# First stretch and routing of a fused attention, expert layer and MLP rebuilt together

## What is computed

```python
# attention, B=2, H=8, S=768, D=64: window |i-j| < 16 and, beside it, 24 block summaries
k_sum = k.reshape(B, H, nb, 32, D).max(axis=3)
v_sum = v.reshape(B, H, nb, 32, D).mean(axis=3)
scores_l = where(|i-j| < 16, q @ k.T / 8, -1e9)
scores_s = q @ k_sum.T / 8 + log(32)
a = softmax(concat(scores_l, scores_s)) ; attn = a @ concat(v, v_sum)
# expert layer on N=1536 rows x of 512: E=8 experts, F=1024, top-1
logits = x/|x| @ (emb/|emb|).T / tau
idx = argmax(logits) ; gate = softmax(logits)[idx]
out[idx == e] = gate * (relu(x @ w1[e]) @ w2[e])
# second layer
h = relu(x @ w_in)            # 512 -> 2048
result = (h * h) @ w_out      # 2048 -> 512
```

## Time and profile before

| | us |
|---|---|
| median of 3 runs | 585.4 (583.68 to 589.5) |
| the profiled execution | 588.62, its span 586.9 |
| PE busy | 539.4 (92% of the span) |
| DVE busy | 282.1 (48%) |
| ACT busy | 231.7 (39%) |
| POOL busy | 113.0 (19%) |
| mean granted clock of TensorE | 0.956 |

### The profile page before, as it was taken

One profiled execution on the slowest core, in us unless ns is written; L12 is line 12 of the kernel. 1 busy time (PEld: TensorE's weight loads), 2 busy tenths in 40 slices (PEclk: granted clock), 3 DMA queues, 4 the chain that ended last, 5 costly groups with the idle time before them and its releaser, 6 DMA issues.

```text
span 586.9 us, 11035 instructions
## 1 busy us (share of the span) xinstructions
PE 539.4 (92%) x4482; PEld 486.2 (83%) x4482; DVE 282.1 (48%) x437; ACT 231.7 (39%) x405; POOL 113.0 (19%) x134
## 2 busy tenths in 40 slices
PE   7498779499999896899999999999999999999997
PEld 6377667498989795889988989989989999998995
DVE  4667757556788494745747223232223223223321
ACT  4568656165564343443654222222122222212221
POOL 8282110111107789520100000000000000000000
PEclk9689988579999998999999999999999999999999
DMA  5877860893729694857721002002002002000000
GB/s 181 200 203 180 194 173 30 267 348 120 251 75 323 227 333 158 282 178 254 250 92 54 1 1 73 0 1 71 0 0 71 0 0 71 0 0 37 1 1 36
DMA packets 62655, 69.50 MB, mean 118 GB/s; under 512 B 22512, under 2 KB 47088, under 8 KB 62232
## 3 DMA queue, kind: packets, MB, share of 16 engines
q1 hardware_dynamic: 59160, 57.36, 31.6%
q0 software_dynamic: 3456, 11.60, 5.6%
HBM read 58.88 MB, written 10.06 MB: 117 GB/s over the span
## 4 chain that ended last, share of the span: by engine, by line
PE 68%; DVE 9%; DMA 9%; POOL 8%; issue 4%; SPq 1%; ACT 1%; POOLq 0%; DVEq 0%
PE psum L881 20%; PE psum L882 20%; PE psum L883 20%; POOL win_lo L522 3%; DMA v_blk<-in_v 2%; POOL win_hi L520 2%; DMA k_raw<-in_k 2%; DMA x_rows_sb<-x_rows,idx_g 1%; DMA win_raw<-in_moe_w_in 1%; DMA x_rows_sb<-x_rows,gather_tab 1%; DVE neg_max L1308 1%; PE psum L708 1%; PE psum L666 1%; DVE wb_lo L1561 1%; PE psum L726 1%
## 5 line engine op out<-in xcount | busy, mean ns | idle before, releaser
L883 PE MATMUL psum<-x_hi,win_lo 128*128 128x256 f32 x384 | 108.7, 283 | 0.0
L882 PE MATMUL psum<-x_lo,win_hi 128*128 128x256 f32 x384 | 108.7, 283 | 0.0
L881 PE MATMUL psum<-x_hi,win_hi 128*128 128x256 f32 x384 | 108.5, 282 | 0.0
L1652 DVE TENSOR_TENSOR h_sq<-h_relu 128x512 f32<-128x512 f32 x48 | 33.2, 691 | 126.6 <-ACT h_relu L1248 126.6
L881 PE MATMUL psum<-wb_hi,h_hi 128*128 128x512 f32 x208 | 83.2, 400 | 0.0
L883 PE MATMUL psum<-wb_hi,h_lo 128*128 128x512 f32 x208 | 81.8, 393 | 0.0
L882 PE MATMUL psum<-wb_lo,h_hi 128*128 128x512 f32 x208 | 81.7, 393 | 0.0
L1248 ACT ACTIVATE h_relu<-psum 128x512 f32<-128x512 f32 x48 | 28.7, 597 | 127.4 <-PE psum L883 127.4
L881 PEld LDWEIGHTS psum<-x_hi,win_hi 128*128 128x128 f32 x384 | 73.6, 192 | 1.4
L882 PEld LDWEIGHTS psum<-x_lo,win_hi 128*128 128x128 f32 x384 | 73.6, 192 | 1.4
L883 PEld LDWEIGHTS psum<-x_hi,win_lo 128*128 128x128 f32 x384 | 73.6, 192 | 0.0
(11 more groups left out here) (199 smaller groups left out, 926.0 us busy)
## 6 DMA issues: line engine op xcount, KB each, us to landing
w_raw<-in_moe_w SPq DMA_DIRECT2D x56, 512.0 KB, 6.1
win_raw<-in_moe_w_in POOLq DMA_DIRECT2D x8, 512.0 KB, 5.2
w_raw<-in_moe_w_out SPq DMA_DIRECT2D x8, 512.0 KB, 5.1
k_raw<-in_k SPq DMA_DIRECT2D x8, 384.0 KB, 3.6
q_raw<-in_q SPq DMA_DIRECT2D x8, 384.0 KB, 5.5
v_blk<-in_v SPq DMA_DIRECT2D x3, 1024.0 KB, 8.0
v_win<-in_v SPq DMA_DIRECT2D x16, 192.0 KB, 3.9
x_rows<-x_all SPq DMA_DIRECT2D x8, 384.0 KB, 4.7
```

The source lines that it names most:

```text
L881: pe.matmul(o, l_hi, r_hi, start=start, stop=False)
L882: pe.matmul(o, l_hi, r_lo, start=False, stop=False)
L883: return pe.matmul(o, l_lo, r_hi, start=False, stop=stop)
L1652: dve.tensor_tensor(h_sq[c % 2][:, :], h_relu[c % 2][:, :], h_relu[c % 2][:, :], ALU.mult)\
```

## The change

1. **Start.** SP loads the embeddings first, and both `load_near` of slots 0 and 1 ahead of the wait for the means; `load_qk(2)` goes behind the means. DVE clears slots 0 and 1 (POOL keeps 2 and 3). Chunk 0 of v is summed by halving, one half of the chunk on DVE and the other on POOL. POOL makes the mask from one band that it copies. The three `fill` of pair 0 go to three PSUM banks, and their filler matmuls (`keep_warm`, 24 in all) are gone. The embeddings are normalised and turned ahead of the first scores.
2. **Pair steps.** `turn_tile` is gone. In the step of pair n, PE turns all six tiles of pair n-1 (`turn_pair`, into the two banks of the turned exponentials), ACT and DVE move a half each, and the second `turn_probs` waits for both. From the step of pair 1 on, DVE regroups k one step earlier. The squares leave the attention.
3. **Routing.** Logits of batch 0 stand between pairs 4 and 5, the comparison in pair 5, the counting in pairs 5 and 6, the placing in pair 6, the list in pair 7. In pairs 6 and 7 ACT moves both halves of the turned exponentials. The norms leave the choice: the largest logit of a row doesn't depend on the row's norm, so `margin` keeps the differences and is scaled in expert block 2. Batch 1 is weighed in the up part of block 0, counted in its down part and placed in the up part of block 1. The 16 filler matmuls ahead of the first `turn_rows` are gone.
4. **w_in.** POOL splits pieces 0, 1, 6 and 7, ACT and DVE split 2 and 3 at the end of block 2, and 4 and 5 at the end of block 3. Gathers 3 and 4 and scatters 1 and 2 no longer stand behind splits on POOL; gather 5, the first of the loop, stands behind the loads and splits of 6 and 7.

The core of the diff (buffers moved in SBUF, renamed semaphores and the removed helpers are left out):

```diff
--- before.py
+++ after.py
+            sp.dma_start(emb_sb[:, :], emb).then_inc(emb_loaded, 16)
             load_qk(0)
             sp.dma_start(v_blk[:, 0, :], v_blocks[:, 0, :]).then_inc(vb_loaded[0], 16)
-            sp.dma_start(emb_sb[:, :], emb).then_inc(emb_loaded, 16)
-            sp.dma_start(tau_sb[:, 0:1], tau.broadcast_to([P, 1])).then_inc(emb_loaded, 16)
-            load_qk(1)
+            sp.dma_start(tau_sb[:, 0:1], tau.broadcast_to([P, 1])).then_inc(tau_loaded, 16)
             sp.wait_ge(zeros_made, 1)
             load_near(0, 0, free=True)
-            load_qk(2)
+            load_qk(1)
+            sp.wait_ge(zeros_made, 2)
+            load_near(0, 1, free=True)
             sp.wait_ge(mean_made, 1)
             sp.dma_start(mean_dram[0:P, :], v_mean[:, 0, :]).then_inc(means_stored[0], 16)
             sp.dma_start(v_blk[:, 1, :], v_blocks[:, 1, :]).then_inc(vb_loaded[1], 16)
             sp.wait_ge(means_stored[0], 16)
             load_means(0, 0)
             load_means(0, 1)
-            load_near(0, 1, free=True)
+            load_qk(2)
             sp.dma_start(v_blk[:, 2, :], v_blocks[:, 2, :]).then_inc(vb_loaded[2], 16)
             load_qk(3)
-            sp.wait_ge(zeros_made, 2)
+            sp.wait_ge(late_zeros_made, 1)
...
+            pool.wait_ge(vb_loaded[0], 16)
+            pool.wait_ge(consts_made, 1)
+            at = BLOCK * D // 2
+            width = at // 2
+            while width >= D:
+                last = pool.tensor_tensor(v_blk[:, 0, at:at + width], v_blk[:, 0, at:at + width],
+                                          v_blk[:, 0, at + width:at + 2 * width], ALU.add)
+                if width > D:
+                    after(last)
+                width //= 2
+            last.then_inc(half_summed, 1)
...
             scatter(0, scatter_tab0)
+            pool.wait_ge(logits_summed, 2)
+            load_win(0)
+            load_win(1)
+            split_win(0, 1)
+            split_win(1, 2)
             pool.wait_ge(x_stored[1], 16 * PAIRS // B)
             pool.wait_ge(routed, 2)
             nblk, final = block_count(pool)
-            load_win(0, 0)
-            load_win(1, 1)
             gather(3, gather_tab)
-            split_win(0)
-            split_win(1)
+            pool.wait_ge(squares_done, NT)
+            load_win(2)
+            load_win(3)
             scatter(1, scatter_tab0)
-            split_win(2)
             gather(4, gather_tab)
-            split_win(3)
-            split_win(4)
+            load_win(4)
+            load_win(5)
             scatter(2, scatter_tab0)
-            split_win(5)
-            split_win(6)
-            split_win(7)
+            load_win(6)
+            load_win(7)
+            split_win(6, 3)
+            split_win(7, 4)
...
+            def turn_pair(pair, bank=4):
+                for half in range(2):
+                    for t in range(GT):
+                        mm = pe.transpose(psum[:, bank + half, t * P:(t + 1) * P], x_all[:, pair, GT * half + t, :],
+                                          ident[:, :])
+                    mm.then_inc(xt_turned, 1)
+            def wait_turned(pairs):
+                pe.wait_ge(xt_moved[0], pairs)
+                pe.wait_ge(xt_moved[1], pairs)
...
+                if pair > 0:
+                    turn_pair(pair - 1)
                 if fills:
                     fill(it + 1, par, 1)
-                if ahead:
-                    scores(*nxt, 1)
+                if pair > 0:
+                    wait_turned(pair)
+                turn_probs(it, par, 1)
+                scores(*nxt, 1)
                 if fills:
                     fill(it + 1, par, 2)
                 values(it, par, 1)
...
-                fill(0, 0, f, first=True)
-                keep_warm(ps_warm, 5)
+                fill(0, 0, f, first=True, bank=(7, 4, 5)[f])
+            pe.wait_ge(emb_normed, 1)
...
+            pair_step(2, 0, True)
+            logits(4)
+            scores(3, 0, 0)
+            pe.wait_ge(logits_moved, 1)
+            turn_probs(2, 1, 0)
+            fill(3, 1, 0)
+            values(2, 1, 0)
+            turn_logits(0, 5)
+            fill(3, 1, 1)
+            pe.wait_ge(logits_read, 1)
+            turn_probs(2, 1, 1)
+            scores(3, 0, 1)
+            fill(3, 1, 2)
+            values(2, 1, 1)
             pe.wait_ge(consts_made, 2)
-            totals(0, 7)
-            values(it, 0, 1)
-            turn_probs(it, 1, 0)
+            totals(0, 5, at=GT * P)
+            turn_pair(4)
+            scores(3, 1, 0)
+            wait_turned(5)
+            pe.wait_ge(totals_moved, 1)
+            turn_probs(3, 0, 0)
             pe.wait_ge(before_made, 1)
+            pe.wait_ge(qk_moved_act, 2 * PAIRS)
             ranks(0, 7)
-            values(it, 1, 0)
-            turn_probs(it, 1, 1)
+            values(3, 0, 0)
...
+            def weigh_second(c):
                 if c == 0:
...
+                    turn_pair(PAIRS - 1, bank=6)
+                elif c == 1:
+                    wait_turned(PAIRS)
+                    logits(6)
+                elif c == 2:
+                    turn_logits(1, 7)
+            def count_second(t, f):
+                if (t, f) == (0, 0):
+                    totals(1, 0)
+                elif (t, f) == (0, 3):
+                    ranks(1, 1)
...
+            def place_second(c):
+                if c == 2:
                     pe.wait_ge(y_moved_dve, 1)
-                    ranks(1, 5)
-            def place_second(t, f):
+                    slots(1, 5)
...
-            keep_warm(psum[:, 3, :], 16)
             turn_rows(0, bank=0)
...
+                if squared is not None:
+                    for t in range(squared, squared + TILES):
+                        squares(t)
+                if win is not None:
+                    win_hi_part(win)
+                    win_hi_part(win + 1)
...
                 scale_out(it, par, 0)
+                if pair > 0:
+                    move_pair(pair - 1)
                 if fills:
                     move_kq(it + 1, par)
                 move_prob(it, par, 1)
                 if fills:
                     key_max(it + 1, par)
-                if ahead:
-                    row_max(*nxt, 1)
-                if tile is not None:
-                    move_tile(tile + 1)
+                if 0 < pair < PAIRS - 3:
+                    regroup_k(*((it + 1, 1) if par == 0 else (it + 2, 0)))
+                row_max(*nxt, 1)
...
+            def move_pair(pair, bank=4):
+                dve.wait_ge(xt_turned, 2 * pair + 2)
+                dve.tensor_copy(x_t1[:, pair % KC, GT * P:2 * GT * P], psum[:, bank + 1, 0:GT * P])\
+                   .then_inc(xt_moved[1], 1)
...
+            def sum_blocks():
+                dve.wait_ge(vb_loaded[0], 16)
+                width = BLOCK * D // 4
+                while width >= D:
+                    link(dve.tensor_tensor(v_blk[:, 0, 0:width], v_blk[:, 0, 0:width], v_blk[:, 0, width:2 * width],
+                                           ALU.add))
+                    width //= 2
+                dve.wait_ge(half_summed, 1)
+                at = BLOCK * D // 2
+                dve.tensor_tensor(v_mean[:, 0, :], v_blk[:, 0, 0:D], v_blk[:, 0, at:at + D], ALU.add)\
+                   .then_inc(mean_made, 1)
...
             regroup_k(0, 0, first=True)
-            move_kq(0, 0, first=True)
+            embeddings()
+            move_kq(0, 0, first=True, bank=4)
             dve.wait_ge(key_zeros_made, 1)
             key_max(0, 0)
+            dve.wait_ge(emb_zeros_made, 1)
+            dve.wait_ge(emb_turned, 1)
+            dve.tensor_copy(emb_t[:, :, 0:E], ps_emb.rearrange("p (c e) -> p c e", e=E)).then_inc(emb_moved, 1)
+            row_max(0, 0, 0)
+            sum_blocks()
+            row_max(0, 0, 1)
             regroup_k(0, 1, first=True)
-            row_max(0, 0, 0)
-            row_max(0, 0, 1)
-            block_means(0)
...
+            choose(0, 5)
+            move_kq(3, 1)
+            move_prob(2, 1, 1)
+            key_max(3, 1)
+            row_max(3, 0, 1)
+            scale_out(2, 1, 1)
+            move_pair(4)
+            move_totals(0, 5, at=GT * P)
+            row_max(3, 1, 0)
             lay_blocks(0, 7)
+            scale_out(3, 0, 0)
             place(0, 7)
+            row_max(3, 1, 1)
             make_hots(0)
-            scale_out(last, 1, 0)
+            scale_out(3, 0, 1)
             list_tokens(0, 7)
-            move_prob(last, 1, 1)
-            scale_out(last, 1, 1)
+            scale_out(3, 1, 0)
...
+            expert(1, behind=place_second)
+            expert(2, behind=lambda c: scale_margins() if c == 0 else None, win=2)
+            expert(3, behind=lambda c: gates() if c == 0 else None, win=4)```

What this makes of the order, at three places. Rows are an engine's instructions in program order, with the line, the operation, the tiles, and in brackets the semaphores that it waits for.

```

(1 more changed line is left out.)

556 lines of the change are left out of this document (261 added, 295 removed).

## The result

The changed kernel takes 568.51 us (median of 4 runs, 567.62 to 569.89) beside 585.87 for the kernel before (median of 4). The ratio is 0.9682, with a 95% interval of 0.9638 to 0.9726: 3.2% faster. The prediction said 557, with a range of 548 to 569. So the sign and the range held, and the likeliest case (552 to 562) did not.

The account below looks back on a forecast made before the run. PE was taken as the bound, with 68% of the chain of waits. Start −5.4, pair steps −14.8 and experts −7.9 sum to −28.1, taking 588.62 to 560.5, or 557 us against the median; range 548 to 569.

Parts of the forecast that it names:

- likeliest case: Whole kernel: a time of 552 to 562 us, with a chance of 0.45.
- Start: From 0 to the first values: they come at 24.0 instead of 29.36, −5.4 us, between −8 and 0.
- The rule's 17.1: Start: if DVE and POOL add in turn on their shared port, the mean is there at 17.1, not 14.2.
- the bound of 0: Start: no gain if k for pair 2, now issued last, holds PE instead.
- Rival 4: Start: it brings nothing, because k of pair 2 or the fills hold PE until 29; +5.4, 562 us; chance 0.06.
- Pair steps: First values to the list of batch 0: 64.25 us instead of 79.06, −14.8, bounded by −8 and −19.
- rival 1: Pair steps: late copies on ACT or DVE keep PE waiting and the clock falls; +10, 567 us; chance 0.17.
- Rival 6: Attention: the lower clock throughout, each of seven steps taking 14.88 instead of 9.2; +40, 597 us; chance 0.03.
- List to first expert matmul: Stretch from batch 0's list to the first expert matmul: 11.8 us as before, a change of 0.
- Rival 5: Before the experts: list early in vain, block 0's first weights not split by 100; at worst 577 us; chance 0.04.
- Experts: Seven expert blocks: 179.3 us against 187.2, −7.9, between −2 and −13.
- Rivals 2 and 3: Experts: gain given back, +8, 565 us, chance 0.14; or gather 5 in time, −7.5, 549 us, chance 0.11.

Follow-up runs that it names:

- e1: Changed kernel with SP issuing k and q of pair 2 right behind the store of the means, ahead of the means' loads; ratio 0.9669 to the kernel before.
- e6: Changed kernel with SP's whole start reordered: k and q of pair 1 ahead of slot 0's near rows, slot 1's near rows last; ratio 0.9651 to the kernel before.
- e7: Changed kernel with ACT, in pair 5's step, regrouping q during the logits and moving k ahead of the exponentials; ratio 0.9663 to the kernel before.
- e9: Changed kernel with DVE's regrouping of k put back to its old place, not one step earlier; ratio 0.9677 to the kernel before.
- e8: Changed kernel with SP issuing the last six of block 0's eight weight loads only when the first gather has landed; 563.8 us, ratio 0.9615.
- e4: Changed kernel with part 4 undone: POOL splits all eight pieces of w_in between its gathers and scatters; ratio 0.9611 to the kernel before.
- e5: Kernel of e4 with POOL starting its loads, gather 3 and splits only when block 1's down part has ended; ratio 0.9775 to the kernel before.
- e10: Changed kernel with the 16 filler matmuls ahead of the first turning of gathered rows put back; ratio 0.9595 to the kernel before.
- e2: Changed kernel with POOL's loads and splits of w_in pieces 6 and 7 moved behind its loop of gathers and scatters; 556.85 us, ratio 0.9474.
- e11: Changed kernel with the edits of e2, e7 and e8, and the last turned pair moved ahead of the first down-weight split; 553.78 us, ratio 0.9443.

## Why the prediction was right in sign and too low by 11.5 us

- **Start** (predicted −5.4, measured −1.5). The term is mis-sized by 3.9. The means were made at 14.80, forecast at 14.2, and two misses cancel in that: DVE began 0.7 earlier than the 12.3 of the working, and its additions took 2.97 instead of 1.8. The rule's 17.1 added both halves at their whole length, which the additions did not take. Three steps failed behind it. "The store adds 3.6 (17.8)" let the store follow at once, and SP was still issuing loads until 17.3. "From which I take 1.3 off" gave no price to the new place of `load_qk(2)`, though the bound of 0 named it. And "three banks for the fills bring that forward" had the scores of pair 1 earlier than before; they ended 2.0 later (25.98), since k of pair 1 is loaded and regrouped later. With SP's order mended the first values came at 26.48 (e1) and 25.80 (e6), so this last step is at least 1.8 of the 3.9. Rival 4 was the nearest case. I had read the queue of the engines and not that of SP.
- **Pair steps** (predicted −14.8, measured −12.4). By the prediction's own sign, a list that is not earlier by 15 or more, its main term was wrong: the list came 13.9 earlier. The steps of pairs 1 to 3 took 25.9 together, where 3 × 8.6 were forecast, but as 8.13, 9.61 and 8.13. In the short ones PE is busy for 8.0, where 8.4 were forecast, and the turned pairs cost no wait: rival 1 fell. In that of pair 2 PE stands idle for 1.36, of which 0.90 have no releaser in the profile. So that sum was right by luck. The 2.4 that lack are mainly in the step of pair 5, 12.33 instead of 9.75, for which the working named no engine: 1.0 is ACT's order (e7), 1.2 the lower clock of that execution. The step of pair 4 took 0.8 more than forecast, the first and the last 1.0 less. The early regrouping of k, which the prediction counted as a gain, brought none (e9). Rival 6 fell: the steps of pairs 1 to 4 ran at 1.00.
- **List to first expert matmul** (predicted 0, measured +0.9). The gather was taken at its old duration. The weights were under way beside it in both kernels; e8 shows that this traffic was worth pricing. Rival 5 fell: PE's wait before the first expert matmul was 0.64 for `x_lo`, as before.
- **Experts** (predicted −7.9, measured −8.1). The sum was right and so was the wait for gather 5 (6 predicted, 6.29 measured, block 4 at 32.0 where 30.8 was forecast). Two misses cancel in that wait: load 6 went out at +93.4 and not at +97.5, and the two splits on POOL took 10.8 (205.34 to 216.13) and not 7.1. The reason for the gain was wrong: part 4 brought nothing by itself (e4), and POOL's earlier start did (e5). The 1.4 for missing fillers was not seen in the profile of e10. Rivals 2 and 3 fell.
- **From the profiled execution to the median.** The prediction took its difference from an execution 3.2 over the median and set it against the median. The change of the profile is compared with another profile, and either lies a few us off its median.

## What to carry to other kernels

A queue that only issues DMAs is an engine with a timeline of its own: before a step is costed at its data's arrival, list what SP still has to issue ahead of it, and which load takes the last place once another is moved forward. Before a stretch is credited to an edit, look at the same stretch in every profile that shares it: here one step took 11.1 or 12.3 us with the same code. When work leaves an engine that is late, ask first what comes last on it behind that work: here one gather behind two splits ate the gain, and its place was worth 8.7 us. A small gather that PE waits for is to be kept apart from large loads that nobody needs yet.

## What the runs showed of the hardware

- A gather of 128 rows of 2 KB reached PE 3.6 us later beside weight loads and stores that e8 holds back, 3.75 MB in all (7.8 against 4.2).
- Four DVE additions took 1.72 us alone and 2.97 beside POOL's, and a regrouping copy 0.56 alone, 1.27 beside a clearing by POOL and 2.08 beside an addition of 2.37. DVE's and POOL's additions went in turn, each ending behind the other engine's by its undisturbed time less 0.07 to 0.16.
- A DMA of short strided rows took SP 3.13 us to issue at 7.60, with a median of 0.65 over the 16 of its line: the queue itself holds up what stands behind it.
- The start differs by 2.15 us between the profiled executions of nine kernels that share it: the first values at 26.98 (e2), 27.58 (e7), 27.88, 28.24 (e4), 29.05 (e10) and 29.13 (e11), with the rest between.
- The same step, with the same order and the same wait of 1.78 on PE, ran at a granted clock of 1.00 in five profiles (11.08 us) and of 0.86 in three (12.3 us).
